# Where the PE's code jumps from one expert to the next, how early the next jump is announced, and a weight split in two parts

## What is computed

```python
def _moe2_ref(x, w_gate, w1, w2, capacity) -> np.ndarray:
    N, D = x.shape
    logits = x @ w_gate
    expert_idx = np.argmax(logits, axis=1)
    ...
    for i in range(N):
        e = expert_idx[i]
        if counts[e] < capacity:
            disp[e, counts[e]] = x[i]
            ...
    h = np.maximum(np.einsum('ecd,edf->ecf', disp, w1), 0.0)
    y = np.einsum('ecf,efd->ecd', h, w2)
    out = np.zeros((N, D), dtype=np.float32)
    for i in range(N):
        if keep[i]:
            out[i] = gate_w[i] * y[expert_idx[i], pos[i]]
```

## Time and profile before

| | |
|---|---|
| median of 3 runs | 529.95 us (529.68 to 533.26) |
| the profiled execution, its own time | 531.95 us |
| its span, first to last instruction | 530.2 us |
| PE busy | 507.9 us, 96% of the span |
| DVE, ACT, POOL busy | 291.2, 239.8, 185.7 us |
| mean granted TensorE clock | 0.996 |

### The profile page before, as it was taken

The page is one execution under the profiler, slowest core; times in us unless marked ns, Lnnn a source line. Parts: engine busy times, 40 slices in busy tenths (PEclk is TensorE's granted clock), DMA queues, the critical chain, the costliest instruction groups (busy, mean ns, idle before and its releaser), DMA issues.

```text
span 530.2 us, 8635 instructions
## 1 busy us (share of the span) xinstructions
PE 507.9 (96%) x3153; PEld 429.7 (81%) x3153; DVE 291.2 (55%) x563; ACT 239.8 (45%) x424; POOL 185.7 (35%) x210
## 2 busy tenths in 40 slices
PE   8999999999999999999999999999998998999993
PEld 7998788888888878888887788897887878888882
DVE  6899664444223343223555654755577778647751
ACT  3899643433222221222443433423356757747620
POOL 2888300000000003000000460053237999998842
PEclk9999999999999999999999999999999999999998
DMA  8987899400000002001222443224695896866100
GB/s 254 253 258 222 292 362 321 129 0 1 1 0 1 2 0 81 0 0 41 79 80 81 159 129 110 81 81 136 213 355 164 321 333 247 314 241 218 44 27 32
DMA packets 28300, 75.08 MB, mean 142 GB/s; under 512 B 5455, under 2 KB 5455, under 8 KB 28240
## 3 DMA queue, kind: packets, MB, share of 16 engines
q1 hardware_dynamic: 24240, 67.97, 39.1%
q0 software_dynamic: 4000, 6.32, 3.3%
HBM read 61.12 MB, written 19.96 MB: 153 GB/s over the span
## 4 chain that ended last, share of the span: by engine, by line
PE 89%; issue 3%; DVE 3%; POOL 1%; DMA 1%; ACT 1%; SPq 0%; POOLq 0%
PE bank L1295 9%; PE bank L1297 9%; PE bank L1296 9%; PE bank L1339 9%; PE bank L1341 8%; PE bank L1340 8%; PE bank L1308 6%; PE bank L1587 3%; PE bank L1260 3%; PE bank L1589 3%; PE bank L1588 3%; PE bank L1585 3%; PE bank L1310 3%; PE bank L1287 2%; PE bank L1451 2%
## 5 line engine op out<-in xcount | busy, mean ns | idle before, releaser
L549 POOL DMA_INDIRECT dispatched_rows<-rows,slot_idx x12 | 14.1, 1172 | 268.6 <-issue 145.4
L367 POOL TENSOR_TENSOR w_lo<-raw,w_hi 128x256 fp32r<-128x256 f32 x100 | 89.5, 928 | 14.1 <-ACT w_hi L351 14.1
L907 DVE SCALAR_TENSOR_TENSOR g<-g,bank 128x512 f32<-128x512 f32 x48 | 33.0, 688 | 107.6 <-ACT g L636 107.6
L636 ACT ACTIVATE g<-bank 128x512 f32<-128x512 f32 x48 | 28.8, 599 | 132.7 <-PE bank L1297 132.7
L351 ACT ACTIVATE w_hi<-raw 128x1024 fp32r<-128x1024 f32 x80 | 82.8, 1052 | 0.0
L367 DVE TENSOR_TENSOR w_lo<-raw,w_hi 128x1024 fp32r<-128x1024 f32 x55 | 72.3, 1314 | 10.1 <-ACT w_hi L351 10.0
L1295 PE MATMUL bank<-x_hi,w_hi 128*128 128x512 f32 x192 | 77.0, 401 | 0.0
L1339 PE MATMUL bank<-w_hi,g_hi 128*128 128x512 f32 x192 | 76.0, 396 | 0.0
L1340 PE MATMUL bank<-w_lo,g_hi 128*128 128x512 f32 x192 | 75.8, 395 | 0.0
L1341 PE MATMUL bank<-w_hi,g_lo 128*128 128x512 f32 x192 | 75.8, 395 | 0.0
L1297 PE MATMUL bank<-x_hi,w_lo 128*128 128x512 f32 x192 | 75.6, 394 | 0.0
(11 more groups left out here) (153 smaller groups left out, 893.5 us busy)
## 6 DMA issues: line engine op xcount, KB each, us to landing
raw<-expert_units SPq DMA_DIRECT2D x64, 512.0 KB, 5.8
raw<-dense_units SPq DMA_DIRECT2D x16, 512.0 KB, 7.1
dispatched_rows<-empty SPq DMA_DIRECT2D x26, 257.0 KB, 11.5
slot_rows<-dispatched_rows SPq DMA_DIRECT2D x26, 257.0 KB, 3.1
tile_in<-attention_tiles SPq DMA_DIRECT2D x12, 384.0 KB, 4.5
tile_in<-attention_tiles SPq DMA_DIRECT2D x12, 336.0 KB, 6.0
queries<-attention_tiles SPq DMA_DIRECT2D x12, 256.0 KB, 4.8
mask<-masks SPq DMA_DIRECT2D x1, 288.0 KB, 5.3
```

Source lines behind the costliest of these rows:

```text
L367: last = engine.tensor_tensor(w_lo[u % RING][:, part], raw[u % RING][:, part], w_hi[u % RING][:, part].bitcast(F32), ALU.subtract)
L907: dve.scalar_tensor_tensor(g32[i % 2][:, :], g32[i % 2][:, :], 1.0, h_bank[i % 2][:, :], ALU.add, ALU.mult).then_inc(s_g, 1)
```

## The change

The jump to the next body is moved behind the first three steps of tile 0's second layer, so that the old body runs steps 0 to 2 of its own tile 0 and the new one steps 3 to 7. In the new body T0 to T3 stand one by one: T0, T1, steps 3 and 4, the announcement of the body after next (before it stood first), T2, step 5, T3, steps 6 and 7. The 192-token bodies begin at instruction 156 of a piece of 256 instead of 120. DVE's weight split inside the hidden steps is made in two halves of 512 columns, behind steps 2 and 4, instead of as a whole behind step 2; POOL's parts stay as they were.

```diff
     PAIRED = P + HALF
-    FIRST_TOKENS, LAST_TOKENS = 1, 4
+    LEAVE_AT = 3
+    REST = [LEAVE_AT, 5, 6, EFT]
...
-    LOW_STEP = 2
+    LOW_STEPS = (2, 4)
...
-    BODY_AT = {P: 0, P + HALF: 120, 2 * P: 80, 2 * P + HALF: 64, 3 * P: 48}
+    BODY_AT = {P: 0, P + HALF: 156, 2 * P: 80, 2 * P + HALF: 64, 3 * P: 48}
...
-        def split_lo(engine, u):
+        def split_lo(engine, u, parts=1, some=None):
+
             engine.wait_ge(s_whi, u + 1)
-            parts = POOL_PARTS if by_pool(u) else 1
-            for n in range(parts):
+            for n in range(parts) if some is None else some:
                 part = slice(n * UC // parts, (n + 1) * UC // parts)
                 last = engine.tensor_tensor(w_lo[u % RING][:, part], raw[u % RING][:, part],
                                             w_hi[u % RING][:, part].bitcast(F32), ALU.subtract)
-            last.then_inc(low_done(u)[0], 1)
+            if some is None or parts - 1 in some:
+                last.then_inc(low_done(u)[0], 1)
...
-                    if e and f == LOW_STEP:
+                    if e and f in LOW_STEPS:
                         for u in splits_of(e)[:1]:
-                            split_lo(dve, u)
+                            split_lo(dve, u, len(LOW_STEPS), (LOW_STEPS.index(f),))
...
-            def tile_outputs(e, j, half, between=lambda f: None):
-
-                if e:
-                    pe.wait_ge(s_orow[j], ROW_STEPS * e)
-                elif j < EARLY_TILES:
-                    pe.wait_ge(s_early_row[j], 1)
-                for f in range(EFT):
+            def tile_outputs(e, j, half, steps=range(EFT)):
+
+                if 0 in steps:
+                    if e:
+                        pe.wait_ge(s_orow[j], ROW_STEPS * e)
+                    elif j < EARLY_TILES:
+                        pe.wait_ge(s_early_row[j], 1)
+                for f in steps:
...
-                def between(f):
-                    if f in (FIRST_TOKENS, LAST_TOKENS):
-                        two_transposes(e, 0 if f == FIRST_TOKENS else 2, w)
-                tile_outputs(e - 1, 0, False, between)
+                announced = None
+                for k in range(KT):
+                    slot_transposes(e, k, w)
+                    if e == 0:
+                        if k % 2:
+                            early_outputs(1, 2 + k // 2)
+                    elif k:
+                        tile_outputs(e - 1, 0, False, range(REST[k - 1], REST[k]))
+                    if k == 1 and e + 1 < E:
+                        announced = announce(e + 1)
+                return announced
 
             def expert(e, w):
-                announced = announce(e + 1) if e + 1 < E else None
-                last_tile(e, w)
+                announced = last_tile(e, w)
...
                 if e + 1 < E:
+                    tile_outputs(e, 0, False, range(LEAVE_AT))
                     go_on(e + 1, announced, f"after{e}_{w}", laid_behind(e, w))
```

More of the change, by code:

```diff
@@ L572, in _ @@
                 if by_pool(u):
-                    split_lo(pool, u)
+                    split_lo(pool, u, POOL_PARTS)
             zeros(NBLK - 1)
@@ L1593, in tile_outputs @@
                         last.then_inc(s_Yupper[j], 1)
-                    between(f)
             def announce(e):
@@ L1644, in go_on @@
                 choose(WIDTHS, name)
-            def two_transposes(e, k, w):
-                slot_transposes(e, k, w)
-                slot_transposes(e, k + 1, w)
             def last_tile(e, w):
-                if e == 0:
-                    two_transposes(e, 0, w)
-                    early_outputs(1, 2)
-                    two_transposes(e, 2, w)
-                    early_outputs(1, 3)
-                    return
-                def between(f):
-                    if f in (FIRST_TOKENS, LAST_TOKENS):
-                        two_transposes(e, 0 if f == FIRST_TOKENS else 2, w)
-                tile_outputs(e - 1, 0, False, between)
+                announced = None
[9 more added lines that the diff above has]
+                return announced
             def expert(e, w):
-                announced = announce(e + 1) if e + 1 < E else None
-                last_tile(e, w)
+                announced = last_tile(e, w)
                 for f in range(EFT):
```

## The result

The changed kernel takes **523.82 us** (median of 6 executions, 523.68 to 524.07) against 531.09 (6 executions, 529.68 to 533.26). The ratio is 0.985, 95% interval 0.9828 to 0.9873: faster by 1.5%. The forecast was 523.7. The three executions of the kernel before that were shown ahead of it had a median of 529.95; with six it is 531.09. So the gain is 7.3 us and not 6.2, and the time came out to 0.1 us because the starting point was 1.1 too low.

The account below looks back on a forecast made before the run. PE's matmul stream plus its standstills bounds the kernel, 10.9 us to win. 5.9 - 1.8 + 2.3 = 6.4, taken as 6.2 from 529.95, gives 523.7; forecast's own range 521.5 to 525.2, with rivals A, B and D to 528.0.

Parts of the forecast that it names:

- (a): At the switches between bodies: nine matmuls queued ahead of the jump hide ordinary switches (4.0 us) and the slow jump; 5.9 us.
- (b): Announcement moved behind the second transposes and two steps of tile 0: its 0.6 to 1.0 us of sequencer time is hidden.
- (c): 192-token bodies start 36 instructions later in their piece, border about two hidden steps earlier: 0 by itself.
- Rival C: The piece border inside the 192-token bodies stalls in hidden step 2: 11 us lost, 534.8; chance 0.06.
- (d): DVE's weight split in halves of 0.80 each: hidden step 5 of experts 1, 2, 3, 4, 6 saves 2.3 of 5.2 us.
- Rival A: DVE halves meet POOL parts and take about 1.1 each, costing as much as the whole: gain 4.0, 526; chance 0.17.
- (e): At the switches, PE waits for DVE's low parts of the slots before hidden step 0: 1.8 us comes back, bounds 0 and 3.2.
- Rivals B and D: B: wait moves to transposes and hidden step 0, 526.3, chance 0.11; D: sequencer stops, switch gaps stay, 527.6, chance 0.05.
- the first rival of the place of the bodies: In the kernel before, bodies at 156 bring the next jump's fetch earlier: jumps 0.3 to 0.4, median falls 1.2 to 1.7.

## Why the prediction was right, and where it was not

**What bounds the kernel**: right. The PE's work stayed at 507.9, and the whole gain is standstill that went.

**(a) The jump behind nine matmuls, 5.9 us**: right in size. At all eight switches the starts are a pitch apart, so the 4.2 of the ordinary switches and the 1.67 of the late jump are gone. Two things in it were not as told. The late jump took 2.30 and not 1.86, and a second one of 2.47 came up. The cover of 2.1 of queue, with the lead of the sequencer, had 0.5 to 0.7 to spare. And the text gave the nine matmuls all but the entry into expert 0: undone one at a time, the two remedies overlap in 2.4 of the 4.2, and only 0.9 of the ordinary switches needs the nine matmuls.

**(b) The announcement, 0**: right at its new place, where it costs nothing. But it isn't a part that only must not hurt: by itself it would take 3.3 of the 4.2 at the ordinary switches, as the nine matmuls would, and it is the only remedy at the entry into expert 0 (0.94).

**(c) The place of the bodies, 0 by itself**: right in the changed kernel (523.66 for 523.82). Rival C, a stall at the border, did not come: in expert 1 hidden steps 1 to 3 start at 382.62, 383.77 and 384.91, which is 1.15 for the four pairs of matmuls of a step and leaves no gap; experts 3, 6 and 7 have none there either.

**(d) The halves, 2.3**: mechanism right, size wrong. In the five bodies the first half took 0.68 to 0.83 (0.80 was taken), and step 5 gained 0.53, 0.71, 0.67, 1.03 and 0.38 in experts 1, 2, 3, 4 and 6, together 3.3. That is the old whole split of the same body less the new first half, each time within 0.03: for expert 4, 1.79 - 0.78 = 1.01 by the two rows

```profile
445.90 1.79 DVE L367 TENSOR_TENSOR w_lo<-raw,w_hi 128x1024 fp32r<-128x1024 f32 x1 [0.25 <-ACT w_hi L351]
```

of the kernel before, and of the changed one

```profile
439.71 0.78 DVE L368 TENSOR_TENSOR w_lo<-raw,w_hi 128x512 fp32r<-128x512 f32 x1 [0.23 <-ACT w_hi L352]
```

The step that failed is "Worked out per body, saved: 0.35 (expert 1), 0.5 (2), 0.5 (3), 0.6 (4, whose split was the longest), 0.35 (6)". It did not use the five durations, and its own 0.80 for a half became 0.70 in it (1.22 - 0.70 = 0.5). The rule beside it (what the split loses in length the PE gains) would have given 3.1 from the five durations in the trace (7.13 less five halves of 0.80). The 0.2 charged to step 7 was a second error: it stood for 0.15, in expert 3 alone. Rival A fell: in these bodies no half took over 0.83. In expert 5, where PE did not stand at step 5 before or after, they took 1.25 and 0.94 beside POOL.

**(e) What comes back, 1.8**: 1.15 came back, at T2 0.22 each in experts 3 and 5, at hidden step 0 0.10, 0.35, 0.10, 0.05 and 0.11 in experts 2 to 6. The step "DVE's chain here hangs on ACT, not on PE, so it doesn't move up" held where the most was expected, at the switch from expert 4 to 5: ACT's copy of T0 began 3.14 behind the old body's last hidden matmul before the change and 3.13 after it. What was mis-sized is a term behind it, the weight split that DVE does between the two pairs of low parts. It was taken as 1.80, from the earlier trace rows, and took 1.26:

```profile
448.43 1.26 DVE L368 TENSOR_TENSOR w_lo<-raw,w_hi 128x1024 fp32r<-128x1024 f32 x1
...
449.62 1.01 DVE L1144 TENSOR_TENSOR e_in<-bank,e_in 128x384 fp32r<-128x384 f32 x2
```

In both kernels the second low parts follow this split without a pause. So of the 1.11 that PE came earlier the shorter split gave 0.54 and the room 0.28, and 0.29 had to come back; 0.27 did, where 0.7 to 0.8 was expected. The same term explains 3 to 4 (split 1.49 before, 1.22 after; 0.3 expected, 0.10 measured) and 2 to 3 (1.32 before, 1.59 after; 0.3 expected, 0.57 measured). At 3 to 4 the other runs bear it out: of the ten profiles with hints and the changed order of PE, six have a split of 1.21 or 1.22 there and lose 0.10 to 0.12 at hidden step 0, one has 1.67 and loses 0.55, and three have 1.81 or 1.82 and lose 0.69 to 0.70. At 1 to 2, 5 to 6 and 6 to 7 the chain did hang on PE in the trace of before (DVE stood 0.15, 0.38 and 0.36 for ACT's second copy, and ACT 0.49 to 0.71 for PE); there 0.4 was expected in all and 0.21 came. The room at hidden step 0 is used up now: the low parts end 0.10 to 0.13 ahead of PE's start in every switch, where it was 0.39 to 0.57.

**The sum**: 5.9 + 3.15 - 1.15 = 7.9 where 6.4 was worked out. The span fell by 8.1; of that, 0.7 was there before the first switch, in a part that the change does not touch, and some 0.5 of the 7.9 went again in pieces under 0.1, at the first hidden step of each body above all.

**From the profile to the median**: "in unprofiled runs the 1.862 us jump may be shorter than here, so I take 6.2" points the right way: the gain is 8.1 between the profiled executions and 7.3 between the medians. What was wrong is the start. The medians of the kernel before over 6, 23, 9 and 11 executions are 531.1, 531.8, 533.3 and 531.5; 529.95, of three, was the low end of a wide scatter. Two errors, a gain 1.1 too small and a start 1.1 too low, cancelled in the predicted time: that it came out to 0.1 is luck, that the gain of 7.3 lies in the forecast's own range of 4.8 to 8.4 is not.

**Rivals B and D** fell: waits at T2 and hidden step 0 are 1.15 in all and not over 3, and no gap is left at a switch.

## What to carry to other kernels

Where a jump's length varies from one execution to the next, put queued work in front of it rather than shorten its mean: the cover takes the mean and the scatter, and a wide scatter of the times can point at a late jump that one profile happens to miss. Where a gap has two remedies, undo each alone before saying which one paid. Price a shorter instruction on an unbroken chain by the old and the new duration at that very place, not by the group's mean; and don't carry the length of an instruction over into the changed kernel where another engine holds it up by turns: the same split took 1.80 before and 1.26 after. Smaller pieces were not cheaper here: quarters lost to halves.

## What the runs showed of the hardware

- After a standstill of the PE of 2.58 us (start to start) the granted clock fell to 0.50, 1.2 GHz, 1.3 us after work had begun again, and stayed there for 3.4 us; it cost 1.3 us on top of a late jump. After one of 1.90 it stayed at 1.00. In the kernel without hints it was 0.50 for 6.8 us from within the standstill of 4.42 on, and for 3.4 us behind one of 3.37, but it stayed at 1.00 behind one of 3.90. So the length of the standstill alone does not tell whether the clock falls.
- DVE's weight splits and POOL's parts hold each other up. At the switch from expert 3 to 4 a split of 1024 columns took 1.22 while the POOL part beside it was stretched to 1.79, and 1.82 in a run where that part took its usual 0.73. One of 256 columns was held 2.58 us by four POOL parts in a row, 0.41 without POOL; one of 1024 columns took 4.58 while five POOL parts went by. The Trainium skill, "SBUF — State Buffer", section "SBUF: two separate sides", says that the loser of the shared port pair fully blocks while the other holds it. The 2.58 agrees, and shows that the loser is not sure of the next turn.
- Hinted jumps out of experts 1 and 3 took from 0.40 to 3.00 us over the profiles, the same code 0.59 in one execution and 2.30 in another; unhinted ones took 3.3 to 6.1, but for the 0.30 into expert 0. With the announcement at the start of the body 2 of 8 of these two jumps were late, with the announcement behind T1 11 of 18, which looks as if a later hint makes a late jump likelier. The two kernels that differ in it alone point the same way, 0 of 2 against 3 of 4 in two profiles, which is too few to show it. The Trainium skill, "Runtime: NRT & Kernel Launch", section "Instruction fetch mechanics", has a taken branch out of the current pages wait for a fetch; the unhinted jumps agree with it.
- The fetches stand in the traces, as packets of 16 KB and about 1 us on the queue "q8 instruction". In all 14 profiles each jump of over 0.45 us from expert 0 on ended 1.35 to 1.52 us after the end of the last such packet: that of 2.30 in the changed kernel at 396.06, its packet at 394.68; that of 1.862 in the kernel before at 398.33, its packet at 396.97. So a hinted jump is late by as much as its packet is. What sets when the packet starts is open. Out of expert 1 it started 1.8 and 2.1 us ahead of the jump in the two kernels with the early announcement and the 192-token bodies at 156, 0.6 ahead and 0.1 behind in the two with them at 120, which speaks for the first rival of the place of the bodies, with one profile each. Without a hint it started 3.5 and 3.6 us into the two longest (5.9 and 6.1) and 0.9 to 1.7 into the others.
